# G for the states of batches 4 to 7 made in batches 1 and 2, attention of batch 0 beside the first sixteen steps

## The chip, the cores and the metric

The kernel runs on one core of one Trainium2 chip. The metric is the device time of one execution in microseconds; three executions of the kernel before took 1258.76, 1259.70 and 1259.81 us, median 1259.7. The profile is of one further execution.

## What is computed

Attention between tokens and states per batch and head gives, per batch, 512 token rows and 32 state rows of 512 features; all go through two feed-forward networks (cut):

```python
def _attn_ref(x, state):           # x 8x8x512x64, state 8x8x32x64
    a = softmax(scale * x @ state.T);  xread = a @ state
    a2 = softmax(scale * state @ x.T); sread = a2 @ x
    return concatenate([xread, sread], axis=2)

def _moe_ref(x, w_in, w_out):      # 4608x512, 512x2048, 2048x512
    h = maximum(x @ w_in, 0.0)
    return h * h @ w_out

def _moe2_ref(x, w1, w2, w3, w_out):
    return (x @ w1) * (x @ w2) @ w3 @ w_out
```

## The kernel before, in words

Every product is done in float32 split in a high and a low part, three matmuls for one (`product`, `passes`). A piece is 128 x 512 of an input (256 KB): SP loads it into one of eight places of `raw`, ACT casts it to its high part, DVE subtracts to get the low part, and `piece_split` counts the pieces that are through. A place of `raw` is loaded again when the piece eight before is through.

For the token rows, attention and the first layer are joined: G = state times w_in is made once per head and batch (`g_dram`), and the hidden layer of a batch is aT times G. The work of PE in order:

1. **The first sixteen steps** (the table `order`, lines 296 to 317). A step k is `("pair", k)` and `("wp", k)`: a pair (`g_pair`) makes G for two heads, four batches' states and 512 columns of w_in, in six matmuls of 64 rows, two at a time side by side; `multiply_w3` adds to the product of w3 and w_out of the second network, twelve full-size matmuls into ps_y. Pairs go to ps_h and ps_t in turn. ACT drains even ones, DVE odd ones (`drain_pair`), SP stores them.
2. **Sixteen more pairs** for the states of batches 4 to 7, with six buffers and three bank pairs, and beside them attention of batch 0 (the table `beside`; `attention_slot` on PE, ACT and DVE, with numbers as of the slots below).
3. **Batches 0 to 7** (`first_block`). A batch has 16 slots f. In a slot PE does h(f) (six matmuls into ps_h), attention of the next batch if the slot has some (slots 3, 4, 12, 13, 15, in ps_t), and y(f - 2) (twelve matmuls into ps_y). ACT and DVE do in slot f, in this order: relu (ACT), square (DVE), in four batches a part of the S sums (`S_part`), the cast of v (ACT) and its low part (DVE), attention of the next batch, the pieces of the slot. In the slots 4 to 11 DVE's attention is two turns, four reductions, two passes over 1024 columns and more; slot 5 has the most.
4. The state rows, then the second network.

Two batches are one turn of a loop on the engines, but batch 0 and the last are written out. The S sums (`S_part`, for the second network) are made in batches 1 to 4, in the tiles `top` and `E_lo`.

Names in rows: t is t1 or t2, s is s1, e is e2; v_hi and v_lo hold the squared hidden layer in the batches. L661 is `product`, L720 is in `g_pair`, L951 is ACT's copy and cast, L1051 its relu, L1207 DVE's subtraction, product or square, L1296 DVE's drain of a pair, L1354 its drain of ps_y.

Of the kernel before, what the change touches and what calls it, by code (L numbers as in the profile page):

```python
# [34 lines left out]
def build_program(nc, x_tok, x_T, state_T, moe_w_in, moe_w_out, moe2_w1, moe2_w2, w3_T, moe2_w_out, out):  # L35
# [11 lines left out]
    BPG = NB // BG  # L47
# [35 lines left out]
    with ctx:  # L83
# [27 lines left out]
        sb("line", [P, 48])  # L111
# [15 lines left out]
        with ExitStack() as start:  # L127
            st_hi = sb("st_hi", [P, 2, 2, NT], F32R, start)
            st_lo = sb("st_lo", [P, 2, 2, NT], F32R, start)
            g_extra = sb("g_extra", [P, 2, 2, C], F32, start)  # L130
# [9 lines left out]
        g_out = [t1[:], t2[:], g_extra[:, 0], g_extra[:, 1], stage[:, 0:2], stage[:, 2:4]]  # L140
# [6 lines left out]
        def st(pairs):  # L147

            if pairs.stop > 2:
                return st_hi[:, pairs.start - 2:pairs.stop - 2], st_lo[:, pairs.start - 2:pairs.stop - 2]  # L150
            return [t[:, 1].rearrange("p c (h t) -> p c h t", h=2)[:, pairs] for t in (aT_hi, aT_lo)]
# [53 lines left out]
        st_zero = sem("st_zero")  # L205
# [11 lines left out]
        g_stored = [sem(f"g_stored{i}") for i in range(6)]  # L217
        g_stored_last = sem("g_stored_last")
# [72 lines left out]
        N_PAIRS = PAIRS * BG * Q  # L291
        HALF = N_PAIRS // BG
        LAST = N_PAIRS - 2

        def step_pieces(k):

            return ([("piece", "w_in", k // Q, k % Q)] + ([("piece", "wout2", k)] if k < KG else [])
                    + [("piece", "w3T", k)])

        order = [("st", 0)] + step_pieces(0)  # L300
        for k in range(HALF):
            order += step_pieces(k + 1) if k + 1 < HALF else []
            order += [("st", k + 1)] if k < 2 else []
            order += [("att", 0)] if k == HALF - PAIRS else []
            order += [("piece", "xT", k - HALF + PAIRS, 0)] if k >= HALF - PAIRS else []
            order += [("pair", k), ("wp", k)]
        order += [("att", 3)]
        beside = {0: [("att", 4)], 1: [("att", 5)], 2: [("att", 6)], 3: [("att", 7), ("piece", "x", 0, 0)],
                  4: [("att", 8), ("piece", "x", 1, 0)], 5: [("att", 9), ("piece", "x", 2, 0)],
                  6: [("att", 10), ("piece", "x", 3, 0)], 7: [("att", 11), ("piece", "G", 0, 0)],  # L310
                  8: [("att", 12), ("piece", "G", 1, 0)], 9: [("att", 13), ("piece", "wout", 0)], 11: [("att", 15)],
                  13: [("piece", "wout", 1)]}
        for k in range(HALF):
            order += [("pair", HALF + k)] + beside.get(k, []) if HALF + k < LAST else []

        def pair_of(p):
            return p % HALF // Q, p // HALF, p % Q

        def pair_banks(p):

            if p < HALF:
                return (ps_h, ps_t)[p % 2][:]
            return (ps_h[:], ps_y[:, 0:2], ps_y[:, 2:4])[(p - HALF) % 3 if p < N_PAIRS - 1 else 1]

        def last_in_banks(p):

            if p < HALF:
                return p - 2
            return p - 2 if p in (HALF, N_PAIRS - 1) else p - 3 if p > HALF + 2 else -1

        def drainer(p):

            return p % 2 if p < HALF else int(p in (HALF + 3, LAST - 1, LAST + 1))
# [6 lines left out]
        def buffer_of(p):  # L340

            k = p - HALF
            return p % 4 if k < 0 else k % 6 if k < 12 else 2 + k % 4
# [19 lines left out]
        tile_slots = slots(KF, **next_x, **own_g, **next_g, **next_tok)  # L363
        g_0 = {1: 2, 2: 3, 4: 4, 5: 5, 6: 6, 7: 7}
# [19 lines left out]
        R_7 = R_1 + (NB - 2) * PT  # L384
        R_S = R_7 + len(flat(tile7_slots))
        N_RING = R_S + len(flat(sread_slots))
        assert 2 * PT % RAW == 0
        number = {p: n for n, p in enumerate(start_pieces)}
        number |= {p: R_0 + n for n, p in enumerate(flat(tile0_slots)) if p[0] == "wout" or p[-1] == 0}
        number |= {p: R_7 + n for n, p in enumerate(flat(tile7_slots)) if p[0] == "w_in_S"}  # L390
        number |= {p: R_S + n for n, p in enumerate(flat(sread_slots))}

        def piece_dst(piece, par):

            kind, k = piece[:2]
            if kind == "w_in":
                k = Q * k + piece[2]
            if kind == "wout2":
                return E_hi[:, k, :], E_lo[:, k, :]
# [11 lines left out]
        def piece_src(piece, b):  # L411
# [3 lines left out]
            if kind == "w_in":  # L415
                return moe_w_in[rows, piece[2] * C:(piece[2] + 1) * C]
# [52 lines left out]
        def store_g(eng, p):  # L469

            c, bg, q = pair_of(p)
            wait_drained(eng, p)
            return eng.dma_start(g_dram[2 * c:2 * c + 2, bg * P:(bg + 1) * P, q * C:(q + 1) * C]
                                 .rearrange("h p f -> p h f"), g_out[buffer_of(p)])
# [5 lines left out]
        def _(sp):  # L480
# [5 lines left out]
            def load_piece(r, piece, b=0, i=0, per_turn=0, n=C):  # L486

                wait_for(sp, piece_split, i * per_turn + r - RAW + 1)
                sp.dma_start(raw[:, r % RAW, 0:n], piece_src(piece, b)[..., 0:n]).then_inc(raw_loaded[r % RAW], 16)

            def tile(b, slot_lists, r0, i=0, kk=None):
                for n, piece in enumerate(flat(slot_lists)):
                    load_piece(r0 + n, piece, b, i, 2 * PT)
                    if kk is not None and n == 3:
                        sp.wait_ge(S_split, i * 2 * KINDS + kk * KINDS + 1)
                        for dst, row, col in ((A11, 0, 0), (A12, 0, 1), (A21, 1, 0), (A22, 1, 1)):
                            sp.dma_start(dst, A_block(i, kk, row, col)).then_inc(A_loaded, 16)
# [4 lines left out]
            for what in [None] + order:  # L502
                if what is not None and what[0] == "pair":
                    store_g(sp, what[1]).then_inc(g_stored[buffer_of(what[1])], 16)
# [3 lines left out]
                while r < min(ring, R_1) and (early[r][0] != "G" or paired >= HALF):  # L508
                    if early[r] == ("G", 0, 0):
                        for i in range(4):  # L510
                            sp.wait_ge(g_stored[i], stored(i, HALF))
# [7 lines left out]
            for i in range(6):  # L519
                sp.wait_ge(g_stored[i], stored(i, LAST))  # L520
            sp.wait_ge(g_stored_last, 16 * 2)
            with sp.Fori(0, (NB - 4) // 2) as i:
                tile(2 * i + 1, tile_slots, R_1, i, 0)
                tile(2 * i + 2, tile_slots, R_1 + PT, i, 1)
            for b in range(NB - 3, NB - 1):
                tile(b, tile_slots, R_1 + (b - 1) * PT)
            tile(7, tile7_slots, R_7)
# [68 lines left out]
        def _(pool):  # L596
            for part in range(3):
                for t in st(st_pairs(part)):
                    last = nc.gpsimd.memset(t.bitcast(F32), 0.0)
                last.then_inc(st_zero, 1)  # L600
# [3 lines left out]
            nc.gpsimd.memset(A11[:, 0:1], 0.0).then_inc(S_split, 1)  # L604
# [12 lines left out]
            for p in range(LAST, N_PAIRS):  # L617
                store_g(pool, p).then_inc(g_stored_last, 16)

# [13 lines left out]
            store_y(0, S)  # L633
            with pool.Fori(0, (NB - 4) // 2) as i:
                for kk in range(2):
                    store_S(i, kk)
                    store_y(2 * i + kk + 1, S)
            for t in range(NB - 3, NB):
# [15 lines left out]
        def _(pe):  # L654
# [48 lines left out]

            def g_pair(p):

                c, bg, q = pair_of(p)
                if p in (0, Q, 2 * Q):
                    pe.wait_ge(st_split, p // Q + 1)
                w_hi, w_lo = st(slice(c, c + 1))
                if p == HALF + 1:  # L710
                    for eng in range(2):
                        pe.wait_ge(wp_drained[eng], 4)
                pe.wait_ge(piece_split, number["w_in", c, q] + 1)
                wait_drained(pe, last_in_banks(p))
                rows = slice(bg * P, (bg + 1) * P)
                x_hi_c, x_lo_c = X_hi[:, Q * c + q, :], X_lo[:, Q * c + q, :]
                for n, (w, m) in enumerate(passes(w_hi, w_lo, x_hi_c, x_lo_c)):
                    for par in range(2):
                        half = head_rows(par)
                        last = nc.tensor.matmul(pair_banks(p)[:, par, :], w[half, 0, par, rows], m[half],  # L720
                                                start=n == 0, stop=n == 2)
# [813 lines left out]
```

## Time and profile before

| | us |
|---|---|
| profiled execution, as a run | 1259.05 |
| its span, first to last instruction | 1257.4 |
| PE busy | 1236.8 (98%) |
| DVE busy | 809.9 (64%) |
| ACT busy | 496.0 (39%) |
| chain that ended last: PE 96%, DMA 3%, DVE 1% | |

Outside the span lie 1.65 us of the run. A busy PE runs at one of two clocks, 2.4 or 1.2 GHz; the granted clock is given as a share of the first, and the mean over the run is 0.992.

### The profile page before, as it was taken

How to read it: one execution, taken by the hardware profiler on the slowest of the kernel's cores; microseconds unless marked ns; L12 is line 12 of the kernel's file. 1: busy time of each engine (PE TensorE's matmuls, PEld its weight loads, DVE VectorE, ACT ScalarE, POOL GpSimd, SP SyncE). 2: the span in 40 equal slices, each digit the busy share in tenths (PEclk: the TensorE clock that was granted, in tenths of full speed). 3: DMA queues.
4: the chain of work that ended last, by engine and by line, in shares of the span. 5: the costliest groups of instructions: out<-in, count | busy, mean ns of one | idle time of the engine just before them, and what ended most of it. 6: DMA issues, size and time to landing. Idle time of an engine off the chain costs nothing.

```text
span 1257.4 us, 19633 instructions
## 1 busy us (share of the span) xinstructions
PE 1236.8 (98%) x7177; PEld 1079.5 (86%) x7177; DVE 809.9 (64%) x1445; ACT 496.0 (39%) x936; POOL 56.6 (5%) x101
## 2 busy tenths in 40 slices
PE   8988999999999999999999999999999999999998
PEld 6656888888888888888889999999999999999998
DVE  6666877678696866667544667575757575757541
ACT  6565565455555555445443422121212121212111
POOL 1000001111011100000000000000000000000000
PEclk9988999999999999999999999999999999999999
DMA  8986444344434322122112950101011010100210
GB/s 296 357 290 240 138 151 163 138 144 161 150 134 157 135 104 93 62 84 67 68 67 79 371 204 1 68 6 62 18 48 33 34 33 33 33 33 0 85 63 22
DMA packets 64632, 139.13 MB, mean 111 GB/s; under 512 B 5696, under 2 KB 6720, under 8 KB 64576
## 3 DMA queue, kind: packets, MB, share of 16 engines
q1 hardware_dynamic: 53984, 100.68, 23.5%
q0 software_dynamic: 10592, 37.75, 8.2%
q8 instruction: 29, 0.48, 0.2%
q14 instruction: 27, 0.22, 0.1%
HBM read 84.93 MB, written 53.48 MB: 110 GB/s over the span
## 4 chain that ended last, share of the span: by engine, by line
PE 96%; DMA 3%; DVE 1%; ACT 0%; issue 0%; SPq 0%; POOL 0%; DVEq 0%; POOLq 0%; ACTq 0%
PE ps_y L661 48%; PE ps_h L661 27%; PE ps_t L661 18%; DMA g_scratch<-g_extra 1%; DMA wp_scratch<-stage 1%; DMA g_scratch<-stage 1%; PE ps_t L720 1%; PE ps_h L720 0%; PE ps_t L685 0%; DMA raw<-in_moe_w_out 0%; DVE v_lo L1207 0%; ACT v_hi L951 0%; DVE t L1207 0%; DVE stage L1318 0%; DVE stage L1296 0%
## 5 line engine op out<-in xcount | busy, mean ns | idle before, releaser
L951 ACT CAST v_hi<-t 128x512 fp32r<-128x512 f32 (+1 forms) x216 | 129.0, 597 | 443.7 <-DVE t L1207 442.8
L661 PE MATMUL ps_y<-v_hi,X_hi 128*128 128x512 f32 (+1 forms) x576 | 219.6, 381 | 3.3 <-DVE stage L1296 3.3
L1207 DVE TENSOR_TENSOR v_lo<-t,v_hi 128x512 fp32r<-128x512 f32 (+1 forms) x216 | 143.0, 662 | 118.7 <-ACT v_hi L951 111.9
L661 PE MATMUL ps_y<-v_hi,X_lo 128*128 128x512 f32 (+1 forms) x576 | 218.1, 379 | 0.0
L661 PE MATMUL ps_y<-v_lo,X_hi 128*128 128x512 f32 (+1 forms) x576 | 218.1, 379 | 0.0
L1207 DVE TENSOR_TENSOR t<-t 128x256 f32<-128x256 f32 (+1 forms) x272 | 143.5, 547 | 101.8 <-ACT t L1051 99.0
L1051 ACT ACTIVATE t<-ps_h 128x512 f32<-128x512 f32 (+1 forms) x144 | 82.5, 573 | 157.4 <-PE ps_h L661 155.8
L661 PEld LDWEIGHTS ps_y<-v_hi,X_hi 128*128 128x128 f32 x576 | 108.8, 189 | 23.0 <-issue 3.7
L661 PEld LDWEIGHTS ps_y<-v_hi,X_lo 128*128 128x128 f32 x576 | 108.7, 189 | 20.4
L661 PEld LDWEIGHTS ps_y<-v_lo,X_hi 128*128 128x128 f32 x576 | 108.9, 189 | 19.5
L1207 DVE TENSOR_TENSOR t<-t,ps_t 128x256 f32<-128x256 f32 (+1 forms) x132 | 72.5, 549 | 47.4 <-PE ps_t L661 33.6
L661 PE MATMUL ps_h<-aT_hi,GA 128*128 128x512 f32 (+1 forms) x288 | 95.7, 378 | 0.5 <-ACT g_extra L951 0.5
L661 PE MATMUL ps_h<-aT_hi,GB 128*128 128x512 f32 (+1 forms) x288 | 95.7, 377 | 0.0
L661 PE MATMUL ps_y<-v_hi,GB 128*128 128x512 f32 (+1 forms) x288 | 91.6, 382 | 0.4 <-DVE v_lo L1207 0.4
L661 PE MATMUL ps_y<-v_hi,GA 128*128 128x512 f32 (+1 forms) x288 | 91.6, 381 | 0.0
L1207 DVE TENSOR_TENSOR t<-t,ps_h 128x256 f32<-128x256 f32 x132 | 54.9, 416 | 55.0 <-PE ps_h L661 42.8
L1207 DVE TENSOR_TENSOR t<-ps_t,t 128x512 f32<-128x512 f32 x64 | 44.2, 690 | 45.5 <-PE ps_t L661 44.7
L951 ACT COPY t<-ps_h 128x256 f32<-128x256 f32 (+1 forms) x74 | 31.5, 426 | 84.7 <-PE ps_h L661 80.8
L661 PEld LDWEIGHTS ps_h<-aT_hi,GA 128*128 128x128 f32 x288 | 53.3, 188 | 11.2 <-ACT g_extra L951 0.9
L661 PEld LDWEIGHTS ps_y<-v_hi,GB 128*128 128x128 f32 x288 | 53.3, 188 | 10.3 <-DVE v_lo L1207 0.6
L1207 DVE TENSOR_TENSOR X_lo<-raw,X_hi 128x512 fp32r<-128x512 f32 x66 | 45.3, 686 | 26.0 <-ACT X_hi L951 25.6
L661 PEld LDWEIGHTS ps_h<-aT_hi,GB 128*128 128x128 f32 x288 | 53.3, 188 | 10.0
(235 smaller groups left out, 2811.2 us busy)
## 6 DMA issues: line engine op xcount, KB each, us to landing
raw<-g_scratch SPq DMA_DIRECT2D x64, 256.0 KB
raw<-in_moe_w_in SPq DMA_DIRECT2D x32, 256.0 KB
raw<-in_x_T SPq DMA_DIRECT2D x32, 256.0 KB
raw<-in_x_tok SPq DMA_DIRECT2D x32, 256.0 KB
y_scratch<-stage POOLq DMA_DIRECT2D x8, 1024.0 KB, 6.2
s_scratch<-top POOLq DMA_DIRECT2D x32, 256.0 KB, 2.5
s_scratch<-E_lo POOLq DMA_DIRECT2D x32, 256.0 KB, 3.5
raw<-y_scratch SPq DMA_DIRECT2D x8, 1024.0 KB, 5.3
```

The costliest lines, as they stand in the source:

```text
L661: mm = nc.tensor.matmul(dst, w, m, start=first and n == 0, stop=last and n == 2)
L720: last = nc.tensor.matmul(pair_banks(p)[:, par, :], w[half, 0, par, rows], m[half], start=n == 0, stop=n == 2)
L951: return nc.scalar.copy(dst, src)
L1051: nc.scalar.activation(t1[:, f % 2, 0:n], ps_h[:, f % 2, 0:n], ACT.Relu).then_inc(relu_done, 1)
L1207: return nc.vector.tensor_tensor(dst, a, b, op)
```

## The change

- The second sixteen pairs leave the start. `order` holds 16 steps only, and attention of batch 0 with the pieces of xT, x, G and w_out for it stands in `beside`, among the steps 1 to 15. Pairs are now taken by column block first (`pair_of`), so that the rows of G that batch 0 needs first are there early.
- ps_t is left to attention in these steps; all pairs go to ps_h, and pair p waits for the drain of pair p - 1.
- The second half of G is made in batches 1 and 2, eight pairs in each: w_in is loaded a second time, one piece per pair (`w_in_again`, split into `top` and `E_lo`), `late_pair` stands in the slots `LATE` between h or attention and y, in both banks of ps_t; ACT drains one bank and DVE the other into `stage` (`drain_late`, last in the slot), POOL stores.
- The split states move into `top` without zeroes around them, so one cast and one subtraction do where two did; three zeroings on POOL go.
- The S sums move from batches 1 to 4 to batches 3 to 6.
- The loops over batches are written out on all engines.

The core of the diff:

```diff
-        N_PAIRS = PAIRS * BG * Q
-        HALF = N_PAIRS // BG
-        LAST = N_PAIRS - 2
+        N_PAIRS = PAIRS * Q
...
+        beside = {1: [("att", 0)], 3: [("piece", "xT", 0, 0), ("piece", "xT", 1, 0)],
+                  4: [("piece", "xT", 2, 0), ("piece", "xT", 3, 0)], 5: [("att", 3)], 6: [("att", 4)], 7: [("att", 5)],
+                  8: [("att", 6)], 9: [("att", 7), ("piece", "x", 0, 0)], 10: [("att", 8), ("piece", "x", 1, 0)],
+                  11: [("att", 9), ("att", 10), ("piece", "x", 2, 0)], 12: [("att", 11), ("piece", "x", 3, 0)],
+                  13: [("att", 12), ("piece", "G", 0, 0)], 14: [("att", 13), ("piece", "G", 1, 0)],
+                  15: [("att", 15), ("piece", "wout", 0), ("piece", "wout", 1)]}
         order = [("st", 0)] + step_pieces(0)
-        for k in range(HALF):
-            order += step_pieces(k + 1) if k + 1 < HALF else []
+        for k in range(N_PAIRS):
+            order += step_pieces(k + 1) if k + 1 < N_PAIRS else []
             order += [("st", k + 1)] if k < 2 else []
...
+            order += beside.get(k, []) + [("pair", k), ("wp", k)]
...
-            return p % HALF // Q, p // HALF, p % Q
...
+            return p % PAIRS, p // PAIRS
...
+        LATE = (5, 6, 7, 8, 9, 10, 11, 14)
+        late_slots = [[pieces + ([("w_in_again", len(LATE) * half + LATE.index(f + 1))] if f + 1 in LATE else [])
+                       for f, pieces in enumerate(tile_slots)] for half in range(2)]
...
+            for t in range(NB):
+                if t in (1, 2):
+                    store_late(t - 1)
+                if 3 <= t < 7:
+                    store_S(*divmod(t - 3, 2))
                 store_y(t, S)
...
+            def multiply_g(banks, c, bg, w_in_hi, w_in_lo):
+
+                cols = slice(bg * P, (bg + 1) * P)
+                for n, (w, m) in enumerate(passes(st_hi[:, c, cols], st_lo[:, c, cols], w_in_hi, w_in_lo)):
                     for par in range(2):
                         half = head_rows(par)
...
+                        last = nc.tensor.matmul(banks[:, par, :], w[half], m[half], start=n == 0, stop=n == 2)
+                return last
...
+                wait_drained(pe, p - 1)
+                multiply_g(ps_h[:], c, 0, *piece_dst(("w_in", p), 0)).then_inc(g_full, 1)
...
+            def late_pair(n, f, a):
+
+                if f == LATE[0]:
+                    pe.wait_ge(att_free[0], uses(a, 0))
+                    pe.wait_ge(att_free[1], uses(a, 1))
+                if f == LATE[-1]:
+                    pe.wait_ge(att_free[0], uses(a, 2))
+                    pe.wait_ge(att_free[1], uses(a, 3))
+                pe.wait_ge(piece_split, number["w_in_again", n] + 1)
+                for drained in late_drained:
+                    wait_for(pe, drained, n)
+                multiply_g(ps_t[:], pair_of(n)[0], 1, *w_in_again[n % 2]).then_inc(late_full, 1)
...
+                def slot(f):
+                    if b in (1, 2) and f in (12, 15):
+                        for drained in late_drained:
+                            pe.wait_ge(drained, len(LATE) * b - (f == 12))
+                    attention_slot(f, b + 1, *ready)
+                    if b in (1, 2) and f in LATE:
+                        late_pair(len(LATE) * (b - 1) + LATE.index(f), f, b + 1)
+                return slot
...
+            def drain_late(n, b):
+                dve.wait_ge(y_stored, 16 * b)
+                wait_for(dve, late_stored[n % 2], 16 * (n // 2))
+                dve.wait_ge(late_full, n + 1)
+                nc.vector.tensor_copy(stage[:, 2 * (n % 2) + 1, :], ps_t[:, 1, :]).then_inc(late_drained[1], 1)
```

How the order stands on the engines, at the three places that the prediction speaks of.

**DVE, batch 1, slot 5.** (t is the square, s and m are attention's, GA a piece of G.) Before:

```order
L1207 TENSOR_TENSOR t<-t 128x512 [waits relu_done]
L1326 REGISTER_ALU
L1207 TENSOR_TENSOR top<-top_f,top 128x512 [waits S_rounded]
L1207 TENSOR_TENSOR v_lo<-t,v_hi 128x512 [waits sq_hi]
L1240 ISA
L1223 STREAM_TRANSPOSE s<-e 128x512 [waits att_free1]
L1243 TENSOR_REDUCE m<-e 128x1
L1244 REGISTER_ALU
L1245 TENSOR_SCALAR m<-m 128x2 [waits max2_done]
L1248 TENSOR_REDUCE m<-s 128x32 [waits s1_ready]
L1211 REGISTER_ALU
L1207 TENSOR_TENSOR GA<-raw,GA 128x512 [waits piece_hi]
```

Now:

```order
L1206 TENSOR_TENSOR t<-t 128x512 [waits relu_done]
L1206 TENSOR_TENSOR v_lo<-t,v_hi 128x512 [waits sq_hi]
L1222 STREAM_TRANSPOSE s<-e 128x512 [waits att_free1]
L1242 TENSOR_REDUCE m<-e 128x1
L1244 TENSOR_SCALAR m<-m 128x2 [waits max2_done]
L1247 TENSOR_REDUCE m<-s 128x32 [waits s1_ready]
L1206 TENSOR_TENSOR GA<-raw,GA 128x512 [waits piece_hi]
L1206 TENSOR_TENSOR E_lo<-raw,top 128x512 [waits piece_hi]
L1357 COPY stage<-ps_t 128x512 [waits late_full,y_stored]
L1206 TENSOR_TENSOR t<-t 128x512 [waits relu_done]
```

The last row is the square of slot 6. The S part is gone; the split of a piece of w_in and the drain of the late pair stand behind the piece of G, ahead of the next square.

**PE, batch 1, slots 6 and 7.** Before there was nothing between h and y of these slots. Now, with a late pair behind the last matmul of h(6):

```order
L659 MATMUL ps_h<-aT_hi,GA 128x512 [waits relu_done]
L659 MATMUL ps_h<-aT_lo,GA 128x512
L659 MATMUL ps_h<-aT_hi,GA 128x512 x2
L659 MATMUL ps_h<-aT_lo,GA 128x512
L659 MATMUL ps_h<-aT_hi,GA 128x512
L708 MATMUL ps_t<-top 128x512 [waits late_drained_dve,late_drained_act,piece_split]
L708 MATMUL ps_t<-top 128x512 x5
L659 MATMUL ps_y<-v_hi,X_hi 128x512 [waits sq_split]
```

The pair waits for both drains of the pair before and for its piece.

**ACT, the first stretch, from the copies of ps_y behind step 7.** Before, with a pair's drain two casts behind the copies:

```order
L951 COPY stage<-ps_y 128x512 [waits wp_full]
L951 COPY stage<-ps_y 128x512
L951 CAST X_hi<-raw 128x512 [waits raw_loaded2]
L951 CAST v_hi<-raw 128x512 [waits raw_loaded3,wp_full]
L951 COPY t<-ps_h 128x1024 [waits g_full,g_stored0]
```

Now:

```order
L954 COPY stage<-ps_y 128x512 [waits wp_full]
L954 COPY stage<-ps_y 128x512
L954 CAST X_hi<-raw 128x512 [waits raw_loaded6,g_full]
L954 CAST v_hi<-raw 128x512 [waits raw_loaded7,wp_full]
L977 ACTIVATE e,d<-e,m 128x512 [waits bias2_done]
L977 ACTIVATE e,d<-e,m 128x512
L954 COPY t<-ps_h 128x1024 [waits g_full,g_stored0]
L954 CAST X_hi<-raw 128x512 [waits raw_loaded0,g_full]
L954 CAST v_hi<-raw 128x512 [waits raw_loaded1,wp_full]
```

The exponentials of attention (e) stand between the casts and the drain of pair 8 (t).

## Rows read from the trace of the kernel before

**Rows 1.** The page: its first line

```profile
span 1257.4 us, 19633 instructions
```

**Rows 2.** Busy time by stretch: us from:to, length, engines, granted clock, DMA share, GB/s

```profile
0.00:71.25 71.25, 67.20 (x297) 46.75 (x298) 43.21 (x65) 38.28 (x66) 6.20 (x16) 0.98 0.88 313
71.25:111.34 40.09, 29.43 (x160) 20.02 (x158) 26.14 (x43) 27.57 (x45) 1.46 (x2) 0.87 0.82 295
111.34:183.93 72.59, 72.50 (x326) 59.98 (x327) 56.72 (x98) 43.56 (x85) 0.72 (x1) 0.98 0.50 158
183.93:255.79 71.86, 71.86 (x333) 59.97 (x332) 53.27 (x91) 39.63 (x75) 9.44 (x17) 1.00 0.43 147
```

**Rows 3.** All engines in order of time (start us, us, operation), second stretch: two drains

```profile
79.69 1.22 DVE L1296 COPY g_extra<-ps_h 128x1024 f32<-128x1024 f32 x1
...
81.05 0.66 PE L720 MATMUL ps_h<-X_hi,aT_hi 64*128 64x512 f32 x2 [1.77 <-DVE g_extra L1296]
...
82.91 1.01 ACT L951 COPY stage<-ps_y 128x1024 f32<-128x1024 f32 x1 [1.53 <-DMA wp_scratch<-stage]
...
84.06 0.80 PE L720 MATMUL ps_y<-X_hi,aT_hi 64*128 64x512 f32 x2 [1.50 <-ACT stage L951]
```

**Rows 4.** Busy time of a short stretch, after a stop

```profile
95.00:98.30 3.30, 3.10 (x14) 3.13 (x15) 0.54 (x1) 1.50 (x2) 0.00 (x0) 0.50 1.06 382
```

**Rows 5.** PE in order of time, last steps of the first stretch

```profile
63.67 0.50 PE L720 MATMUL ps_h<-X_hi,st_hi 64*128 64x512 f32 x2
...
67.51 0.50 PE L720 MATMUL ps_t<-X_hi,st_hi 64*128 64x512 f32 x2
...
71.25 0.39 PE L661 MATMUL ps_t<-x_hi,bd_hi 128*128 128x512 f32 x1
```

**Rows 6.** PE in order of time, slot 5 of batch 1: h, y, next h

```profile
198.89 0.39 PE L661 MATMUL ps_h<-aT_hi,GA 128*128 128x512 f32 x1
...
200.25 0.39 PE L661 MATMUL ps_y<-v_hi,X_hi 128*128 128x512 f32 x1
...
202.97 0.39 PE L661 MATMUL ps_h<-aT_hi,GA 128*128 128x512 f32 x1
```

**Rows 7.** ACT in order of time, slot 6 of batch 1: exponentials, and what follows

```profile
207.54 0.72 ACT L974 ACTIVATE e<-e,m 128x512 f32<-128x512 f32 x1
...
208.25 0.71 ACT L974 ACTIVATE e<-e,m 128x512 f32<-128x512 f32 x1
...
208.96 0.61 ACT L951 CAST GA<-raw 128x512 fp32r<-128x512 f32 x1
```

**Rows 8.** DVE in order of time, batch 1, slots 1, 5, 6 and 8

```profile
184.13 1.29 DVE L1354 COPY stage<-ps_y 128x512 f32<-128x512 f32 x2
...
201.08 0.69 DVE L1207 TENSOR_TENSOR t<-t 128x512 f32<-128x512 f32 x1 [2.12 <-ACT t L1051]
...
202.52 0.69 DVE L1207 TENSOR_TENSOR v_lo<-t,v_hi 128x512 fp32r<-128x512 f32 x1
203.13 0.70 DVE L1223 STREAM_TRANSPOSE s<-e 128x512 uint32<-128x512 uint32 x1
...
205.64 0.68 DVE L1207 TENSOR_TENSOR GA<-raw,GA 128x512 fp32r<-128x512 f32 x1
206.24 0.68 DVE L1207 TENSOR_TENSOR t<-t 128x512 f32<-128x512 f32 x1
...
208.27 1.22 DVE L1207 TENSOR_TENSOR s<-s,m 128x1024 f32<-128x1024 f32 x1
...
215.76 1.21 DVE L1259 TENSOR_REDUCE d<-s 128x32 f32<-128x1024 f32 x1
...
217.49 0.63 DVE L1207 TENSOR_TENSOR x_lo<-raw,x_hi 128x512 fp32r<-128x512 f32 x1
```

**Rows 9.** PE in order of time, second stretch: pairs in a row

```profile
75.98 0.39 PE L720 MATMUL ps_y<-X_hi,aT_hi 64*128 64x512 f32 x2
...
76.67 0.40 PE L720 MATMUL ps_h<-X_hi,aT_hi 64*128 64x512 f32 x2
```

More of the change, by code:

```diff
@@ L145, in G @@
             return half[:, k % (Q * HG // 2), 0, :], half[:, k % (Q * HG // 2), 1, :]
[L147 to L151, printed above, removed]
+        st_hi, st_lo = (top[:, k:k + 2].rearrange("p a (b t) -> p (a b) t", t=NT) for k in (0, 2))
+        w_in_again = [(top[:, 4], top[:, 5]), (top[:, 6], E_lo[:, 6])]
         def sr(a):
@@ L507, in _ @@
                     ring += 1
[L508 to L511, printed above, removed]
+                while r < min(ring, R_1) and (early[r][0] != "G" or paired > last_pair(early[r])):
+                    if early[r][0] == "G":
+                        for p in (last_pair(early[r]) - 1, last_pair(early[r])):
+                            sp.wait_ge(g_stored[buffer_of(p)], stored(buffer_of(p), p + 1))
                     load_piece(r, early[r])
@@ L517, in _ @@
             for r in range(r, R_1):
-                load_piece(r, early[r])
[L519 to L527, printed above, removed]
+                if early[r][0] == "G" and not early[r][2]:
+                    for p in (last_pair(early[r]) - 1, last_pair(early[r])):
+                        sp.wait_ge(g_stored[buffer_of(p)], stored(buffer_of(p), p + 1))
+                if early[r] == ("G", 0, 1):
+                    for i in range(4):
+                        sp.wait_ge(g_stored[i], stored(i, N_PAIRS))
+                load_piece(r, early[r])
+            for b in range(1, NB - 1):
+                tile(b)
+            for n, piece in enumerate(flat(tile7_slots)):
+                load_piece(R_7 + n, piece, 7)
             for n, piece in enumerate(flat(sread_slots)):
@@ L718, in g_pair @@
                     for par in range(2):
                         half = head_rows(par)
[L720 to L722 removed]
+                        last = nc.tensor.matmul(banks[:, par, :], w[half], m[half], start=n == 0, stop=n == 2)
+                return last
+            def g_pair(p):
+                c, q = pair_of(p)
+                if p < 3:
+                    pe.wait_ge(st_split, p + 1)
+                pe.wait_ge(piece_split, number["w_in", p] + 1)
+                wait_drained(pe, p - 1)
+                multiply_g(ps_h[:], c, 0, *piece_dst(("w_in", p), 0)).then_inc(g_full, 1)
@@ L1007, in _ @@
                     act.wait_ge(st_loaded[what[1]], 16)
-                    act.wait_ge(st_zero, what[1] + 1)
-                    for h in range(2):
-                        last = copy(st(pairs)[0][head_rows(h), :, h, :], stT[head_rows(h), pairs, :])
-                    last.then_inc(st_rounded, 1)
+                    copy(st_hi[:, pairs, :], stT[:, pairs, :]).then_inc(st_rounded, 1)
                 if what[0] == "att":
```

309 lines of the change are left out of this document (126 added, 183 removed).

## The prediction

> **What bounds the kernel now.** I read the page first, then the stretches, then PE's order of time, then DVE's. The profiled execution spans 1257.4 us [rows 1] (1259.05 us as a run, against a median of 1259.7); all times below are made against that execution. The stretches [rows 2] show three regimes. In the first 71.25 us PE is busy for 67.20. In the next 40.09 us, where G of batches 4 to 7 is made beside attention of batch 0, PE is busy for 29.43 only, at a mean clock of 0.87. From 111.34 on PE is never free: a batch takes 71.86 us, all busy. So time can be won only in the 40 us, and any matmul put into a batch costs its full length. What of the 40 us is lost is seen in two stops [rows 3]: PE waits 1.77 us for a drain by DVE and 1.50 us for one by ACT. Idle adds up to 40.09 - 29.43 = 10.7 us, and the half clock costs more (0.50 from 95.0 to 98.3 us, after a stop of over 2 us) [rows 4].
>
> **Removed.** The second stretch vanishes as a stretch. Its contents go to two places: attention of batch 0 into the 16 steps, the second 16 pairs into batches 1 and 2.
>
> **The first stretch grows.** A step is 67.51 - 63.67 = 3.84 us [rows 5], and there are still 16, so without waits the last product with w3 ends where it did, at 71.25. Attention of a batch on PE is what a batch of 71.86 has beyond its 16 slots of h (1.36 us) and y (2.72 us) [rows 6]: 71.86 - 16 x 4.08 = 6.6 us. That gives 77.8. Then waits, since all pairs now share the banks of ps_h and pair p+1 needs the drain of pair p. Between a pair and the next there are 3.84 us. A drain costs 84.06 - 82.91 = 1.15 us on ACT and 81.05 - 79.69 = 1.36 on DVE until PE goes on [rows 3], so alone it fits; but it stands in its engine's queue. Pair 8 is drained by ACT behind two copies of ps_y, two casts and the two exponentials of attention: about 1.0 + 1.0 + 1.4 us (the two exponentials run from 207.54 to 208.96 [rows 7]; a cast or copy of 512 columns I estimate at 0.5, somewhat under DVE's 0.60 to 0.65 [rows 8]), then 1.15 + 0.1, together 4.65 after wp 7 ends, and PE is back after 3.84: a wait of 0.8. Pair 11's drain by DVE stands behind six splits (3.6), the sums (1.7), two passes over 1024 columns (1.1 and 1.2) and takes 1.3: 8.9 us for two steps of 7.7, a wait of 1.2. Laying both queues out so for all steps I get 0.5 before pair 2, 0.8 before pair 9, 0.5 before pair 10 and 1.2 before pair 12, 3.0 us, and then 1.5 before h(0) (DVE has sread's turn, two splits and the last drain in front). y(0) follows h(0), h(1), h(2) and a wait of 0.4: 77.8 + 3.0 + 1.5 + 4.1 + 0.4 = 86.8 us, where it was 111.34. Behind y(0) both engines are later against PE than before, with seven pieces in a row to split; h(4) waits 1.6 us for G. Before, batch 0 took 72.59 us from y(0) to h(2) of batch 1, some 2.1 of it at the half clock; now 70.5 + 1.6. I add 1.5 us of half clock, less than before because the stops are shorter. h(2) of batch 1 then starts at 86.8 + 70.5 + 1.6 + 1.5 = 160.4 instead of 183.93: **23.5 us won**. Bounds: no wait and no half clock at all gives 8.0 more (31.5); PE idle and half clock as in the old second stretch (10.7 idle instead of my 6.5, 4 us of half clock instead of 1.5) gives 16.8.
>
> DMA: the 16 steps take 1 MB of xT more in steps 3 and 4 and 1 MB of x in 9 to 12, and the stretch moved 313 GB/s at a share of 0.88 before [rows 2]. The order of SP puts xT eight pieces ahead; I cost it at the 0.5 us before pair 2, and at up to 3 us if the ring is late.
>
> **Batches 1 and 2 grow.** Eight pairs each, as the order shows, one per slot in slots 5 to 11 and one in 14, between h(f) and y(f - 2).
> 1. PE. A pair between full-size products costs its step less twelve matmuls of 0.227: 3.84 - 2.72 = 1.12 us [rows 5, 6]. Pairs in a row cost 76.67 - 75.98 = 0.69 [rows 9]. The new ones all stand alone, so 1.12: 9.0 us a batch, 17.9 in both.
> 2. The drain. Each late pair is written to the same two banks of ps_t, so PE may begin it only when DVE has drained the one before, and that drain stands last in DVE's slot. In slot 5 of batch 1, h starts at 198.89 and DVE's square at 201.08, the split of v at 202.52, the attention part runs from 203.13 to 205.64 and the split of G to 206.24 [rows 6, 8]. The S part between square and split fills a wait for ACT, so taking it away brings nothing forward. Now come the split of w_in (0.60) and the drain (half of 1.29: 0.65) [rows 8], and 0.14 until PE sees it: 207.63. PE gets there at 198.89 + 1.36 (h) + 1.12 (pair) + 2.72 (y) + 1.36 (h) = 205.45. **PE waits 2.2 us**, once in each of the two batches.
> 3. The other slots. PE comes back every 5.20 us. DVE needs 1.44 (square to split of v) + 0.60 + attention + 0.60 + 0.60 + 0.65, so 3.9 plus attention: 1.1 to 1.2 in slots 6, 9 and 10 (1024 columns each, busy for 1.22), 1.7 in 8 [rows 8], and some 0.9 in 7 (two tiny operations and a wait for ACT, my estimate). Where PE has just waited, DVE goes straight on and 5.1 fits in 5.20; where it has not, DVE starts its slot 0.8 late and 0.9 is waited. Before the pairs of slots 7 to 11 that makes 0.0, 0.5, 0.9, 0.0 and 0.9. The pair of slot 14 waits 0.3 for its piece. With the 2.2 that is 4.8 us a batch.
> 4. A batch grows by 9.0 + 4.8 = 13.8, both by **27.6 us**. The half clock after the 2.2 us costs little here, since PE is the one that waits; I add 1.0 for both.
> Bounds: 17.9 if no drain holds PE, and 32 if PE is at the half clock for 3 us in each of three places.
>
> **At nothing.** The S part moves from batches 1 to 4 to batches 3 to 6; batch 1 with it and the rest run at 71.86 [rows 2], so batches 5 and 6, which gain it, stay so. ACT's new casts and copies (eight of each per batch) stand in front of DVE's and are done earlier. POOL's stores of late pairs have two slots, 10 us, until their half of stage is needed. SP's wait for the last late store stands before G of batch 4, needed five slots on; behind it are only pieces of batch 3 of which the first six are through. The loops are written out on every engine; batch 0 was already written out and PE was never idle for instructions in it. Fewer memsets at the start are off the path.
>
> **Sum.** 27.6 + 1.0 - 23.5 = +5.1 us: 1259.05 + 5.1, **1264.2 us**, 0.4% slower. A measurement here tells 0.2%, 2.5 us, from no change.
>
> **Rule and rows.** The isolated pair costs 1.12 against 0.69 in a row; that is what the Trainium skill, "TensorEngine Tiling (Array Packing)", Key Properties, says: a change of the tiling mode drains the engine. By that rule the trace agrees, and the rule speaks against this change, which leaves every pair between full-size products. At 0.69 each the sixteen late pairs would be 11.0 us instead of 17.9, and the sum -1.8 us. The same page of the Trainium skill, PSUM Bottleneck, says that tiling speeds the matmuls but not the evacuation of PSUM, and that both ScalarE and VectorE should share it. They do share it here; no row of this trace shows a late drain, so the rule only stands beside item 2.
>
> **Rivals.**
> - The drain does not hold PE (faster). Decides if DVE ends slot 5 within 6.6 us of h's start instead of 8.7. The traced order of slot 5 speaks against it (7.35 us without the two new operations), that PE never waited for DVE in a batch speaks for it. Then 17.9 - 23.5 = -5.6: 1253.5. Chance 0.12.
> - The half clock sets in. Stops of 1.77 and 1.50 us were followed by low clock [rows 2, 4], and a batch has one of 2.2 and three of 0.5 to 0.9. Up to 4 us more: 1268.5. Chance 0.15.
> - The first stretch starves: xT late, or ACT and DVE, which hand attention to each other in turn, behind by a step. 5 us more: 1269. Chance 0.10.
> - The queues are shorter than I laid them out, and the first stretch has no waits: 6 us less, 1258. Chance 0.05.
> - That G's second half is not moved is no case: the order shows it.
>
> **The numbers.** My forecast has 0.58; its own range is 1260.5 to 1267.5. A quarter of it and the last rival fall within 0.2%, 1257.2 to 1262.2. Faster 0.12, same 0.20, slower 0.68. The range of 1257.5 to 1269.5 leaves out the first rival and a little above.
>
> **To be seen.** In the profile after: y(0) of batch 0 near 87 us; h(2) of batch 1 near 160; batches 1 and 2 at 85 to 86 us each, the others at 71.9; among PE's waits, L708 for "DVE stage L1357", the longest in each batch about 2.2 us, some 9 us in all. Wrong would be: no such wait (then the first rival), a batch 1 beyond 88 us (the clock), or y(0) later than 91.

## The result, and the profile after

The changed kernel takes 1262.4 us (median of 20 executions, 1260.8 to 1264.5), the kernel before 1258.9 (20 executions, 1256.9 to 1260.1). The ratio is 1.0027 with a 95% interval of 1.0020 to 1.0034: slower by 0.27%. The forecast was 1264.2 with a range of 1257.5 to 1269.5, and slower with 0.68. A second run of the same kernel (e9 below) took 1261.3 us against 1258.9, 2.4 us more; why the two runs differ by 1.1 us is told there.

The profiled execution of the changed kernel took 1263.78 us with a span of 1262.2, 4.8 more than [rows 1]. The stretches, cut at y(0) of batch 0 (85.55) and at h(2) of batches 1, 2, 3 and 4 (columns as in rows 2):

```profile
0.00:71.25 71.25, 64.14 (x292) 45.16 (x293) 54.97 (x86) 45.46 (x80) 2.60 (x10) 1.00 0.92 323
71.25:85.55 14.30, 13.04 (x69) 10.29 (x68) 6.62 (x14) 4.83 (x10) 0.75 (x1) 1.00 0.60 218
85.55:158.54 72.99, 71.12 (x327) 58.77 (x327) 58.24 (x102) 45.26 (x90) 0.00 (x0) 1.00 0.44 136
158.54:245.53 86.99, 82.78 (x382) 64.68 (x381) 56.34 (x95) 43.78 (x83) 6.46 (x9) 0.98 0.41 133
245.53:332.40 86.87, 82.67 (x382) 64.51 (x380) 56.35 (x95) 43.78 (x83) 6.48 (x9) 0.98 0.43 143
332.40:404.26 71.86, 71.86 (x333) 59.98 (x332) 53.48 (x91) 39.63 (x75) 9.38 (x17) 1.00 0.44 152
```

Beside [rows 2]: h(2) of batch 1 starts at 158.54 instead of 183.93, 25.4 us earlier. Batches 1 and 2 take 86.99 and 86.87 us instead of 71.86, 30.1 us more. Batch 3, which now also holds the S part, takes 71.86 as before. 30.1 - 25.4 = 4.7 of the 4.8 us are in these three numbers; from h(2) of batch 4 to the end both profiles take 857.9 us. In each of the two grown batches 4.2 us are idle (86.99 - 82.78), where PE never waited before.

PE's waits (us in total, times, longest us):

```profile
PE ps_t L708 <- DVE stage L1357: 7.9, 8, 2.1
PE ps_h L708 <- ACT t L954: 2.0, 2, 1.3
...
PE ps_h L708 <- DVE t L1293: 1.5, 2, 1.1
```

The first line is new in kind: the late pair (L708, into ps_t) waits for DVE's copy of the pair before (L1357, into stage), four times in a batch. (The fifth, 0.26 us in slot 14, is listed under "issue".) How the longest of them comes about is seen in the chain of waits through slots 5 and 6 of batch 1 (start us, us, what):

```profile
175.69 0.70 DVE t L1206
...
176.47 0.63 ACT v_hi L954
...
177.12 0.69 DVE v_lo L1206
177.81 0.62 DVE s L1222
...
179.12 1.21 DVE m L1247
180.33 0.60 DVE GA L1206
180.93 0.60 DVE E_lo L1206
181.53 0.61 DVE stage L1357
182.14 0.14 issue
182.28 0.96 PE ps_t L708 x6
183.24 4.54 PE ps_y L659 x12
```

From 175.69 to 182.14 the chain runs over DVE, with ACT's cast of v (v_hi) in between: square, split of v, the attention part, the split of G, the split of w_in, the drain, and only then does PE go on. That is the queue that the prediction laid out. What it held to be small is in the next row: y, twelve matmuls, takes 4.54 us, where it took 2.72 [rows 6]. PE's own rows say why (start us, us, operation):

```profile
182.28 0.50 PE L708 MATMUL ps_t<-top 64*128 64x512 f32 x2 [2.06 <-DVE stage L1357]
...
184.05 0.63 PE L659 MATMUL ps_y<-v_hi,X_hi 128*128 128x512 f32 x1
184.48 0.63 PE L659 MATMUL ps_y<-v_lo,X_hi 128*128 128x512 f32 x1
...
187.38 0.39 PE L659 MATMUL ps_y<-v_hi,X_lo 128*128 128x512 f32 x1
```

From 184.05 on the matmuls stand 0.43 us apart instead of 0.23: that is the lower of the clock's two levels, 1.2 GHz against 2.4, until about 187.

### The profile page after: what moved, and what is told of

It reads as the page before. It is cut to its first block, busy times and chain, and to the rows that moved or that the text cites. A ratio compares the mean times of both kernels' runs of the same rounds, so it can differ in the third digit from the quotient of the medians.

```text
span 1262.2 us, 18860 instructions
## 1 busy us (share of the span) xinstructions
PE 1237.7 (98%) x7177; PEld 1076.3 (85%) x7177; DVE 824.1 (65%) x1471; ACT 498.6 (40%) x952; POOL 62.8 (5%) x109
## 4 chain that ended last, share of the span: by engine, by line
PE 89%; DVE 6%; ACT 2%; issue 1%; DMA 0%; SPq 0%; POOL 0%; DVEq 0%; ACTq 0%; POOLq 0%
PE ps_y L659 43%; PE ps_h L659 25%; PE ps_t L659 19%; DVE v_lo L1206 1%; ACT v_hi L954 1%; DVE t L1206 1%; PE ps_t L708 1%; DVE X_lo L1206 1%; PE ps_h L708 1%; PE ps_t L683 0%; DMA raw<-in_w_T 0%; ACT t L1049 0%; DVE x_lo L1206 0%; DVE GA L1206 0%; DVE d L1258 0%
## 5 line engine op out<-in xcount | busy, mean ns | idle before, releaser
L1206 DVE TENSOR_TENSOR X_lo<-raw,X_hi 128x512 fp32r<-128x512 f32 x74 | 50.4, 688 | 21.9 <-ACT X_hi L954 21.3
```

The lines of the kernel that those rows point to most:

```text
L1206: return nc.vector.tensor_tensor(dst, a, b, op)
```

## The experiments

Eleven runs were made, nine of them of new kernels; e9 and e10 repeat the changed kernel and e3. The gauge in what follows is the time from the start of h(6) to the start of h(7) in batch 1: 5.20 us without any wait (4.08 + 1.12), 8.91 in the changed kernel (2.06 of stop, 0.06 that each stop costs beside its length, the rest half clock).

**e1: the drain is taken out of the end of the slot.** On ACT and on DVE:

```diff
@@ in_slot of batch_slot @@
-                    if b in (1, 2) and f in LATE:
-                        drain_late(len(LATE) * (b - 1) + LATE.index(f), b)
@@ h_chunk: of ACT behind relu, of DVE behind the square @@
+                if t in (1, 2) and n == S and f in LATE:
+                    drain_late(len(LATE) * (t - 1) + LATE.index(f), t)
```

> Both halves of each late drain stand ahead of the cast and the split of v in their slot, instead of last in it; nothing else moves. Queue theory (PE waits for whatever stands last in DVE's slot; a lone pair costs 1.12 us whatever happens): the drain fills the 0.8 us that DVE waits for ACT's cast between square and split, but the split of the w_in piece is now last, so the stop before the pair of slot 6 falls from 2.06 to about 1.5 us and is charged to the split of the piece, not to the drain; some 1 us less per batch, 2 us in all: about 1260.4 us. Rival 1 (the drain itself is what PE waits for, and once it is out of the way the pairs wait for nothing): 4.2 us of waits and 1.4 us of half clock less per batch, 11 us in all: 1251. Rival 2 (the stop is a fixed latency between a late pair and the next, whatever the order of DVE's queue): 1262.4, waits as they were.

Measured 1257.9 us (0.9991 of before, 0.9982 to 1.0000). Batches 1 and 2 take 83.84 us each. PE's waits:

```profile
PE ps_t L708 <- DVE E_lo L1206: 2.8, 2, 1.4
...
PE ps_t L708 <- DVE top L1206: 1.5, 4, 0.6
```

The wait moved to the split of w_in, and the longest is 1.4 us, as the queue theory had it; the rival in which only the drain matters is out. But 4.5 us were won, not 2. The half clock behind the late pairs is gone too: behind the 1.4 us the gauge reads 6.66 = 5.20 + 1.4 + 0.06. Without half clock the changed kernel's batch is 85.38 us (e3 below shows it), so e1's order itself saves 1.5 a batch, 3.0 in both; the rest fits the 1.0 to 1.3 us that the half clock costs in an average execution (worked out under e9 to e11).

**e2: drain and w_in piece both early.** On top of e1 the piece for the next late pair comes first in its slot's list, and ACT and DVE split it ahead of the attention part:

```diff
@@ slots, and with them SP's loads @@
-    late_slots = [[pieces + ([("w_in_again", len(LATE) * half + LATE.index(f + 1))] if f + 1 in LATE else [])
+    late_slots = [[([("w_in_again", len(LATE) * half + LATE.index(f + 1))] if f + 1 in LATE else []) + pieces
@@ in_slot, shown for DVE @@
-                    attention_slot(f, b + 1, 1 - b % 2)
                     for n, piece in enumerate(slots_of[b][f]):
+                        if n == 0 and piece[0] != "w_in_again":
+                            attention_slot(f, b + 1, 1 - b % 2)
                         split_piece(first_piece[b] + len(flat(slots_of[b][:f])) + n, piece, 0)
+                        if piece[0] == "w_in_again":
+                            attention_slot(f, b + 1, 1 - b % 2)
+                    if not slots_of[b][f]:
+                        attention_slot(f, b + 1, 1 - b % 2)
```

> As the kernel before it in this series (drain ahead of the split of v), and the split of the w_in piece for the next late pair stands ahead of the attention part of its slot instead of behind everything. Queue theory: DVE is done with both, counted from the square, after 0.6 + 0.65 + 0.6 + 0.6 = 2.5 us, long before PE comes back after 5.2: no wait before any late pair, so no half clock behind one: 4.2 + 1.4 us less per batch, 11.2 us in all: 1251.2 us, batches 1 and 2 at 81.0 us each (71.9 and eight pairs at 1.12), which is faster than the kernel before the change (1258.9). Rival (fixed latency, or DMA of the w_in pieces late): batches 1 and 2 stay at 85 to 87 us, 1260 to 1262 us. Second rival (the lone pair's 0.43 us above a pair in a row are themselves waits for DVE): batches 1 and 2 at 71.9 + 8 x 0.69 = 77.4, 1244 us.

Measured 1251.9 us (0.9944, 0.9931 to 0.9958). DVE in slot 6 of batch 1 (square, drain, split of v, split of w_in), and the stretches of batch 1 and batch 3 (batch 2 takes 80.80 us too):

```profile
181.51 0.69 DVE L1211 TENSOR_TENSOR t<-t 128x512 f32<-128x512 f32 x1
182.11 0.68 DVE L1364 COPY stage<-ps_t 128x512 f32<-128x512 f32 x1
182.94 0.69 DVE L1211 TENSOR_TENSOR v_lo<-t,v_hi 128x512 fp32r<-128x512 f32 x1
183.54 0.68 DVE L1211 TENSOR_TENSOR top<-raw,top 128x512 fp32r<-128x512 f32 x1
```

```profile
158.57:239.37 80.80, 80.80 (x381) 63.24 (x380) 56.33 (x95) 43.92 (x83) 6.48 (x9) 1.00 0.44 143
...
320.17:392.04 71.87, 71.87 (x333) 59.97 (x332) 53.48 (x91) 39.65 (x75) 9.39 (x17) 1.00 0.42 147
```

PE is busy throughout, and the drain fits in the time in which DVE waited for ACT's cast. A batch grows by 80.80 - 71.87 = 8.93, eight lone pairs at 1.12. DVE does the same work, in another order.

**e3: the pair first, in the first stretch.**

```diff
-            order += beside.get(k, []) + [("pair", k), ("wp", k)]
+            order += [("pair", k)] + beside.get(k, []) + [("wp", k)]
```

> In the first stretch the pair of a step comes ahead of the attention part and the pieces that stand beside it, on every engine, so its drain is no longer behind them in ACT's and DVE's queues; batches as in the changed kernel. Queue theory: the waits before pairs 2, 9, 10 and 12 (1.06, 0.73, 0.41, 1.12 us) and most of that before h(0) (0.97) go, y(0) comes 3.5 to 4.8 us earlier, at about 81.5 instead of 85.85, and the whole at about 1258.5 us. Rival (the pieces of w_in, w3T, xT and x are late from DMA, so that the steps wait for them instead): waits for a piece's split take their place, y(0) within 1 us of where it was, 1262 us.

Measured 1257.7 us (0.9986, 0.9977 to 0.9995), and as e10, once more, 1257.8 (0.9989, 0.9978 to 1.0000). The waits before pairs 9, 10, 12 and h(0) are gone, the one before pair 2 is down to 0.26; the one before pair 1 stays, at 1.58 (1.55 in e10). y(0) starts at 82.93 in this profile, where a wait of 1.64 before pair 6 was new, and at 80.97 in e10's, where it was not. ACT's row says where the new one comes from (start us, us, operation):

```profile
32.42 0.62 ACT L954 CAST v_hi<-raw 128x512 fp32r<-128x512 f32 x1 [1.63 <-DMA raw<-in_w_T]
```

The cast of a piece of w3 waits 1.63 us for its transfer, DVE's split waits for the cast, and DVE's drain of pair 5 stands behind the split. In e10 the same cast starts at 30.38 without a wait. So the theory holds, and it covers this wait too: even with the pair first, its drain stands behind the pieces of the step before, and when a transfer is late PE waits for the drain.

**e4: the orders of e2 and e3 together.**

> The orders of e2 and e3 together. If both costs are independent waits in queues, the gains add: 1262.4 - 11.2 - 4.0 = 1247.2 us, 12 us faster than the kernel before the change, whose place it would take. If the gain of the first stretch is given back behind it (batch 0 waits for its pieces or for G read back), it is as e2: 1251.

Measured 1247.2 us (0.9907, 0.9892 to 0.9922), the value expected. y(0) starts at 81.48, both batches take 80.80. The gains add; this version beats the kernel before by 12 us and the changed one by 15.

**e5: every late pair twice, in the changed kernel.**

```diff
+                multiply_g(ps_t[:], pair_of(n)[0], 1, *w_in_again[n % 2])
                 multiply_g(ps_t[:], pair_of(n)[0], 1, *w_in_again[n % 2]).then_inc(late_full, 1)
```

> The changed kernel with the six matmuls of every late pair issued twice (the second set starts the sums anew, so the result is the same): 96 matmuls more on PE, in a row behind the first six. Queue theory: a second set costs 0.69 us, the step of pairs in a row, eight of them 5.5 us a batch; but they fill time in which PE waited (4.2 us of waits in a batch, each shortened by up to 0.69), and the stop of 2.06 shrinks to about 1.4, after which e1 shows no half clock; a batch grows by 2 to 3.4 us, from 86.9 to about 89 to 90, both by 4 to 7: 1266.4 to 1269.2 us. Rival (the waits come at a fixed time after the pair, so more matmuls push everything back): 11 us more, 1273.4, waits as they were.

Measured 1268.25 us (1.0072, 1.0054 to 1.0090). A batch takes 88.91 us, 3.5 over the 85.38 without half clock, for 5.5 us of added matmuls; no half clock followed its stops. Two waits are left besides that of slot 14, in slot 6 and slot 9:

```profile
183.19 0.50 PE L708 MATMUL ps_t<-top 64*128 64x512 f32 x2 [1.36 <-DVE stage L1358]
...
201.46 1.65 PE L708 MATMUL ps_t<-top 64*128 64x512 f32 x12 [0.53 <-DVE stage L1358]
```

So the waits end at a time that DVE sets, and matmuls put ahead of them fill them.

**e6: the same in e4, where nothing waits.**

> e4 with the six matmuls of every late pair issued twice, the same edit as e5, where no late pair waits. If the 1.12 us of a lone pair are 0.69 of matmuls and 0.43 paid once for going into the 64-row tiles and out again, a late slot grows from 5.20 to 5.89 us and the kernel by 16 x 0.69 = 11.0 to 1258.3. If a pair costs 1.12 each time beside full-size work (slower matmuls, weight loads not hidden), the slot is 6.32 and the kernel 1265.1.

Measured 1258.2 us, 11.0 over e4. A late slot takes 5.89 us: the second set costs 0.69. **e7: e4 with the late pairs over all 128 rows.** Both banks then hold the sum over two heads, so this kernel leaves out the true G of batches 4 to 7; the matmuls, waits and transfers are as many.

```diff
-                        half = head_rows(par)
+                        half = slice(0, P) if bg else head_rows(par)
```

> e4 with the late pairs' matmuls taken over all 128 rows instead of the 64 of one head (both banks then hold the sum of two heads, so G of batches 4 to 7 is another quantity; counts, columns, waits and transfers are unchanged). If the 0.43 us belong to the tiles, six full-size matmuls cost their 6 x 0.227 = 1.36 us and a late slot 5.44: e4 + 16 x 0.24 = 3.9 us, 1251.1, and the tiles save only 0.24 of the 0.67 us that half the matmul time would. If the 0.43 us are paid for any work put between h and y (another bank, another stationary), the slot is 4.08 + 1.36 + 0.43 = 5.87 us: 1257.9.

Measured 1251.0 us, 3.8 over e4; a late slot takes 5.44. The last matmul of h, the pair and the first two of y, in e2 (64 rows) and in e7 (128 rows):

```profile
179.87 0.39 PE L659 MATMUL ps_h<-aT_hi,GA 128*128 128x512 f32 x1
180.19 0.50 PE L708 MATMUL ps_t<-top 64*128 64x512 f32 x2
180.52 0.40 PE L708 MATMUL ps_t<-E_lo,top 64*128 64x512 f32 x2
180.76 0.39 PE L708 MATMUL ps_t<-top 64*128 64x512 f32 x2
181.08 0.50 PE L659 MATMUL ps_y<-v_hi,X_hi 128*128 128x512 f32 x1
181.41 0.40 PE L659 MATMUL ps_y<-v_lo,X_hi 128*128 128x512 f32 x1
```

```profile
170.13 0.39 PE L659 MATMUL ps_h<-aT_hi,GA 128*128 128x512 f32 x1
170.36 1.52 PE L708 MATMUL ps_t<-top 128*128 128x512 f32 x6
171.72 0.39 PE L659 MATMUL ps_y<-v_hi,X_hi 128*128 128x512 f32 x1
171.95 0.39 PE L659 MATMUL ps_y<-v_lo,X_hi 128*128 128x512 f32 x1
```

In e7 every step is 0.23, over the borders too. In e2 the steps at the borders are longer: 0.32 from h into the pair, 0.33 to its second two, 0.32 into y, 0.33 to y's second, each about 0.1 over the 0.23, together 0.4 of the 0.43.

**e8: the drain one place earlier only**, behind the attention part and ahead of the two splits.

> The changed kernel with each late drain moved one place only, ahead of the two splits that end its slot instead of behind them. Queue theory: what PE waits for is the last of DVE's three operations, now the split of the w_in piece, and it ends when the drain ended; the stops keep their places and lengths within 0.2 us (2.0 before slot 6) and are charged to the split: 1262.4, within 1 us. Rival (the drain is what matters): as it ends up to 1.3 us earlier, the stop shrinks to 0.8 and 6 to 8 us are won, 1255.

Measured 1261.8 us (1.0022). The stops stay (1.96 and 1.97 the longest), and are charged to the splits:

```profile
PE ps_t L708 <- DVE E_lo L1206: 4.3, 4, 2.0
PE ps_t L708 <- DVE top L1206: 3.0, 4, 0.9
```

**e9 to e11: the half clock.** e3's first profile had the changed kernel's batches with the same stops of 2.06, but no half clock (gauge 7.33, batches of 85.38 and 85.35 us). So the changed kernel ran again, e3 ran again, and e3 ran with h(8) and h(9) of batch 0 multiplied twice, to make the stops come later:

```diff
-                for k in range(kc):
+                for k in list(range(kc)) * (2 if isinstance(t, int) and t == 0 and f in (8, 9) else 1):
```

> The changed kernel once more, for a second profile of it. In its first profile both stops of 2.06 us were followed by a stretch at half clock (1.65 and 1.6 us lost); in that of e3, whose batches are the same to the row, the same two stops of 2.06 were followed by none. If the clock's answer belongs to the kernel (what PE did before the stop, in the same order each time), this profile has both stretches again, a span near 1262, and h of slot 7 in batch 1 comes 8.9 us after h of slot 6. If it is chance in each execution, one or both may be missing: span 1259 or 1260.5, and 7.3 us between the two.

> e3 once more. If the clock's answer belongs to the kernel: no half clock behind its stops again (7.3 us from h of slot 6 to h of slot 7 in both batches), span 1256 to 1257. If it is chance: 8.9 us in one or both batches, span up to 1260.

> e3 with h of slots 8 and 9 of batch 0 multiplied twice (the second time starts the sums anew, so the result is the same): 12 matmuls of 0.227 us, 2.7 us more, so that the stops in batches 1 and 2 fall at 180.4 and 265.8 us from the start instead of 177.6 and 263.0, near where those of the changed kernel lie, and nothing else differs. If it is only when the stop comes that decides on the half clock, it returns in both batches: e3's time plus 2.7 plus 3.2, 1263.5. If not, e3 plus 2.7: 1260.4.

e9 measured 1261.3 us (1.0017, 1.0006 to 1.0029; span of the profile 1260.8), e10 1257.8, e11 1259.9. In e9, ten us around each of the two stops:

```profile
180.00:190.00 10.00, 7.94 (x32) 5.31 (x30) 6.70 (x11) 4.75 (x10) 1.43 (x2) 0.83 0.56 159
...
265.00:275.00 10.00, 7.94 (x39) 5.81 (x39) 8.51 (x13) 5.18 (x12) 0.78 (x2) 1.00 0.36 102
```

The gauge reads 8.86 in batch 1 and 7.33 in batch 2: the half clock came behind one stop of 2.06 us and not behind the other. In e10 it is 8.82 and 7.35, in e11 7.34 and 7.33. So the kernel's order does not decide alone. Nor does the time from the start: the changed kernel's second stop begins at 267.20 us in its first profile and at 267.31 in e9's, and only the first was followed by half clock.

e11 takes 2.1 us more than e10, not 5.9: 2.7 were added, and 0.64 came back at the last attention part of batch 0, whose slot is 6.98 us instead of 7.62. But it did not move the stops as meant. They begin at 178.05 and 263.40 us, only 0.4 to 0.5 later than in e3's profile (177.59 and 262.97), since e3's wait before pair 6 is missing too. Whether it matters in which place of the kernel's time a stop falls was therefore not tried.

Over the profiles of the four kernels with a stop of 1.96 to 2.06 us (changed, e3, e8 and e11, six profiles, twelve stops) the half clock followed six times and cost 1.5 to 1.6 us each. It followed none of the stops of 1.36 to 1.47 us behind y(0) in these kernels, in e1 and in e5. Shorter stops are not safe for all that: in e4 and e11 the granted clock is 0.53 and 0.50 from 8.5 to 11.5 us, behind a stop of 1.22 and one of 0.66 or 0.42, and before the change it fell right behind the stop of 1.77 [rows 3] (0.62 from 81 to 82 us).

Only one execution of each run has a profile, but the mean granted clock is on record for every execution. In the twelve profiles since the change it is 0.999 or 1.000 without a half-clock stretch, 0.997 or 0.998 with one and 0.996 with two. By that measure:

- Of the changed kernel's 28 executions (both runs) the 12 with 0.999 took 1260.7 to 1261.6 us, mean 1261.05, and the 16 with less took 1262.0 to 1264.5. The half clock costs 1.3 us in the mean of the first 20 and 1.0 in that of all 28. In the first run 6 of 20 were without it, in e9 6 of 8, which is why the medians differ.
- A clock below 0.999 had 24 of 38 executions with the changed order of the first stretch (changed, e9, e8) and 17 of 27 with the pair first (e3, e10, e11), the same share, though in the profiles it was five stops of six and one of six. In the kernels whose batches have no stop of 2 us (e1, e2, e4 to e7) it was 4 of 34.

So most of the half clock comes with the stops of some 2 us in batches 1 and 2, and whether it comes in a given execution looks like chance. The mean clock does not say where in an execution it fell. The Trainium skill, "TensorE: Matmul & The Clock Gate", Part 1, says that what watches the engine's activity runs freely and does not start anew with a kernel, so that when the clock changes varies from run to run. The traces agree with that rule, as the two stops at 267.2 us show, but do not test it.

## Why the prediction was right, and where it was off

**The sign and its reason: right.** The change buys 25.4 us at the start and pays 30.1 in two batches. The forecast was 23.5 and 27.6 + 1.0.

**The first stretch.** y(0) was forecast for 86.8 and starts at 85.55. PE's waits there:

```profile
12.08 0.50 PE L708 MATMUL ps_h<-X_hi,top 64*128 64x512 f32 x2 [1.26 <-ACT t L954]
...
17.03 0.50 PE L708 MATMUL ps_h<-X_hi,top 64*128 64x512 f32 x2 [1.06 <-DVE t L1293]
...
47.46 0.51 PE L708 MATMUL ps_h<-X_hi,top 64*128 64x512 f32 x2 [0.73 <-ACT t L954]
...
51.83 0.50 PE L708 MATMUL ps_h<-X_hi,top 64*128 64x512 f32 x2 [0.41 <-DVE t L1293]
...
60.69 0.50 PE L708 MATMUL ps_h<-X_hi,top 64*128 64x512 f32 x2 [1.12 <-DVE g_extra L1293]
...
80.88 0.50 PE L659 MATMUL ps_h<-aT_hi,GA 128*128 128x512 f32 x1 [0.97 <-DVE g_extra L1293]
...
91.35 0.47 PE L659 MATMUL ps_t<-x_hi,bd_hi 128*128 128x512 f32 x1 [1.44 <-issue]
```

(The row at 12.08 is pair 1, 17.03 pair 2, the next three are pairs 9, 10 and 12, then h(0) and attention part 3.) Pairs 9, 10 and 12 waited 0.73, 0.41 and 1.12 us, forecast 0.8, 0.5 and 1.2; h(0) 0.97 for 1.5, y(0) 0.29 for 0.4; pair 2 waited 1.06 for 0.5. Pair 1 was missed: it now shares its banks with pair 0, whose drain by ACT stood behind casts that waited for a transfer:

```profile
8.79 1.28 ACT L954 CAST X_hi<-raw 128x512 fp32r<-128x512 f32 x2 [1.78 <-DMA raw<-in_moe_w_in]
...
10.93 1.00 ACT L954 COPY t<-ps_h 128x1024 f32<-128x1024 f32 x1
```

That makes the waits 5.8 us in sum where 4.9 were forecast. Yet y(0) came 1.25 us earlier. Two things of the base ran the other way, and I had taken both over: its half clock (the mean clock in the first 71.25 us is 1.00 now and was 0.98 [rows 2], 0.02 x 71.25 = 1.4 us), and idle that the new waits replace (idle in those 71.25 us grew from 4.05 to 7.11, by 3.1, for 4.6 us of waits before pairs). Together they are 2.9 us and a little more than enough.

Behind y(0) I had 1.6 us before h(4) and 1.5 of half clock. The stop came, at 1.44 us, from the cause that the prediction names, seven pieces in a row to split, but already before attention part 3 at 91.35. The view charges it to "issue"; DVE's row shows what it waited for, the split of the last two pieces of xT, which ends at 91.25:

```profile
89.96 1.29 DVE L1206 TENSOR_TENSOR x_lo<-raw,x_hi 128x512 fp32r<-128x512 f32 x2
```

The half clock did not come. Even so this part is only 0.6 us shorter than forecast (72.99 for 73.6), because its base of 70.5 was too low: the half clock before the change cost about 1.7 us there (granted clock 0.50 from 112 to 115 us, 0.94 to 118) and not 2.1, and the last attention part, with a wait of 0.43 at 144.69, takes 7.64 us where later batches take 6.98. With y(0) 1.25 earlier, h(2) of batch 1 is 1.9 us earlier than forecast. Misses of both signs met here.

**The late pairs: right.** 1.12 each was forecast, and e2 shows 8.93 for eight. e6 and e7 split it: 0.69 for the matmuls and 0.43 once for the change of tiles. The Trainium skill, "TensorEngine Tiling (Array Packing)", Key Properties, says that a change of mode drains the engine. The runs agree: without a change of mode (e7) the 0.43 us are not there, and they are paid once however many tiled matmuls stand together (e6). They show the price and where it is paid; that it is a drain of the engine no run shows by itself. Alone between full-size products the tiles save 1.36 - 1.12 = 0.24 us of six matmuls, where in a row they save 0.67.

**The drain: right.** Forecast 2.2 us before slot 6's pair, 0.0, 0.5, 0.9, 0.0 and 0.9 before those of slots 7 to 11, 0.3 in slot 14, 4.8 in all; the profile has 2.06, 0, 0.41, 0.74, 0, 0.74 and 0.26, 4.2. The forecast's rival that the drain does not hold PE is refuted. e8 and e1 make the name more exact: PE waits for both the drain and the split of w_in, and what holds it is whichever DVE does last, the split as soon as the drain moves.

**The half clock: the reason wrong, the size near by luck.** The term was "I add 1.0 for both", with the reason that it costs little here since PE is the one that waits. The reason failed: the two stretches cost 8.91 - 5.20 - 2.06 = 1.65 and 1.6 us, 3.2 in the profiled execution, although PE had just waited. The size came out near because the half clock is often missing: on average it costs 1.0 to 1.3 us. It is to be forecast as a spread of 0, 1.6 or 3.2 us, not as a rival that happens or not. In the profiled execution 2.2 us more half clock and 0.6 of restarts behind waits (5.52 us for slot 14, where 5.20 and a wait of 0.26 make 5.46) stood against 1.2 us less waiting and 1.9 more won at the start, so that +4.8 came out where +5.1 was forecast. That the sum came so near in this execution is luck in part. The medians differ by 3.5, and by 2.4 in e9. (4 us on top of 1264.2 are 1268.2; the prediction's half-clock rival has 1268.5. Nothing hangs on it.)

**Costed at nothing: right.** Batch 3 with the S part takes 71.86, the loops written out brought no wait for instructions, and the stores of late pairs held nobody.

## What to carry to other kernels

An operation that another engine waits for belongs where its data come ready, not last in the slot where it was convenient to write: the same DVE work in another order saved 4.6 us a batch, and with the same done in the first stretch a change that lost 3.5 us wins 12. When one such operation is moved, look at once at what stands last in its place; moving the drain by one place gained nothing, moving it to the front without the split gained a third of what both gained. And half-row matmuls put singly between full-size ones pay for the change of tiles: take them from a trace where they stand alone, not from a row of them.

## What the runs showed of the hardware that was not expected

- The clock's fall behind a stop of some 2 us is not fixed by the kernel. The same stop of 2.06 us was followed by half clock in one batch and not in the next of the same execution (e9), six times in twelve over six profiles, 1.5 to 1.6 us each. One profile can therefore mislead by 3 us here, as much as the effect that was measured. What decides it in an execution stays open.
- The price of going from full-size matmuls to 64-row tiles and back is spread over four steps of about 0.1 us each: two into the tiles, two out of them, 0.4 of the 0.43 in all, and it does not grow with the number of tiled matmuls (e6).
- The mean granted clock of an execution, a single number, goes with whether such a stretch was in it: 0.999 against 0.998 or less split the changed kernel's 28 executions at 1261.8 us without an overlap.
